# Token tiles loaded from ScalarE's queue, padding issued by two engines, and the last stage's turning and splitting moved to other steps

## What is computed

```python
# stage 1: attention with a threshold, 4 x 8 heads, 576 tokens, head size 64
scores = scale * q @ k.T
scores = where(scores >= max(scores) - tau, scores, -1e9)
x = softmax(scores) @ v                       # 2304 tokens x 512
# stage 2: each token goes to one of 8 experts
logits = x @ w_gate + modality_bias[modality_id]
e = argmax(logits);  gate = softmax(logits)[e]
x = gate * (relu(x @ w1[e]) @ w2[e])          # 512 -> 1024 -> 512
# stage 3: one dense layer with mish
h = x @ w_in                                  # 512 -> 2048
out = (h * tanh(softplus(h))) @ w_out         # 2048 -> 512
```

## Time and profile before

| | |
|---|---|
| median of 3 runs | 1046.27 us (1044.63 to 1048.16) |
| profiled execution: its own time, its span | 1049.75 us, 1048.1 us |
| mean granted clock of TensorE | 0.974 of full |
| PE, PEld, DVE busy | 981.8, 825.5, 673.2 us |
| ACT, POOL busy | 503.7, 466.1 us |
| stage 1 and routing | 0 to about 356 us |
| stage 2 | 356 to 610 us |
| stage 3 | 610 to 1048 us |

### The profile page before, as it was taken

The page is one execution under the profiler, slowest core; times in us unless marked ns, Lnnn a source line. Parts: engine busy times, 40 slices in busy tenths (PEclk is TensorE's granted clock), DMA queues, the critical chain, the costliest instruction groups (busy, mean ns, idle before and its releaser), DMA issues.

```text
span 1048.1 us, 17884 instructions
## 1 busy us (share of the span) xinstructions
PE 981.8 (94%) x6304; PEld 825.5 (79%) x6305; DVE 673.2 (64%) x1200; ACT 503.7 (48%) x952; POOL 466.1 (44%) x558
## 2 busy tenths in 40 slices
PE   6999999999995399999999779999999999999995
PEld 4878877878874288888887668888889888889894
DVE  5788788788785321111115068988879878888773
ACT  3666666666662122222225155554545455545542
POOL 3222235633232663000000027767777777777774
PEclk9999999999998599999999899999999999999998
DMA  2111126122111762111112440000101000000000
GB/s 88 62 51 59 54 90 238 49 90 82 44 50 47 247 206 70 50 40 47 43 40 62 158 121 1 31 1 31 31 31 31 1 31 1 11 21 1 31 1 31
DMA packets 41849, 62.19 MB, mean 59 GB/s; under 512 B 27825, under 2 KB 27825, under 8 KB 41009
## 3 DMA queue, kind: packets, MB, share of 16 engines
q1 hardware_dynamic: 35744, 39.69, 12.2%
q0 software_dynamic: 4480, 18.42, 4.9%
q10 hardware_dynamic: 1552, 3.15, 0.9%
HBM read 43.86 MB, written 17.39 MB: 58 GB/s over the span
## 4 chain that ended last, share of the span: by engine, by line
PE 84%; DVE 6%; DMA 2%; issue 2%; ACT 2%; ACTq 1%; SPq 1%; POOL 1%; POOLq 0%; DVEq 0%
PE psum L369 6%; PE psum L1136 6%; PE psum L1121 6%; PE psum L1119 6%; PE psum L1138 5%; PE psum L1137 5%; PE psum L1120 5%; PE psum L341 4%; DVE rr L1210 3%; PE psum L869 3%; PE psum L845 3%; PE psum L871 3%; PE psum L870 3%; PE psum L847 3%; PE psum L846 3%; PE psum L345 3%
## 5 line engine op out<-in xcount | busy, mean ns | idle before, releaser
L1210 DVE RECIPROCAL rr<-rr 128x384 f32<-128x384 f32 x96 | 244.0, 2542 | 0.9 <-ACT rr L1164 0.9
L1072 POOL TENSOR_TENSOR uu<-uu,ex 128x384 f32<-128x384 f32 x96 | 97.5, 1015 | 291.6 <-ACT uu L1158 291.5
L433 ACT ACTIVATE prob<-ssb,smin 128x576 f32<-128x576 f32 x144 | 111.7, 777 | 112.3 <-DVE ssb L519 112.3
L519 DVE TENSOR_SCALAR_CACHE_REDUCE ssb<-psum,tauk 128x576 f32<-128x576 f32 x144 | 112.7, 816 | 54.6 <-PE psum L328 47.3
L1119 PE MATMUL psum<-x2T_hi,w_in_hi 128*128 128x384 f32 x384 | 132.4, 345 | 5.9 <-DVE gg L1216 3.6
L254 POOL TENSOR_TENSOR limit<-smin,margin 128x2 f32<-128x2 f32 (+1 forms) x80 | 58.2, 727 | 169.3 <-DVE ssb L519 169.1
L1121 PE MATMUL psum<-x2T_hi,w_in_lo 128*128 128x384 f32 x384 | 130.6, 340 | 0.0
L1120 PE MATMUL psum<-x2T_lo,w_in_hi 128*128 128x384 f32 x384 | 130.0, 338 | 0.0
L948 DVE TENSOR_TENSOR hT_lo<-psum,hT_hi 128x512 fp32r<-128x512 f32 x38 | 26.3, 691 | 160.3 <-ACT hT_hi L899 160.3
L1136 PE MATMUL psum<-w_hi,g_hi 128*128 128x512 f32 x288 | 114.7, 398 | 4.3 <-ACT osb L1187 2.5
L1138 PE MATMUL psum<-w_hi,g_lo 128*128 128x512 f32 x288 | 113.8, 395 | 0.0
(11 more groups left out here) (188 smaller groups left out, 2236.2 us busy)
## 6 DMA issues: line engine op xcount, KB each, us to landing
qk<-in_qk_dram SPq DMA_DIRECT2D x16, 640.0 KB, 4.0
vsb<-in_v_dram SPq DMA_DIRECT2D x16, 384.0 KB, 3.3
xrow<-xs SPq DMA_DIRECT2D x21, 256.0 KB, 3.0
ys<-ysb SPq DMA_DIRECT2D x19, 257.0 KB, 3.0
stage<-in_w_in_dram POOLq DMA_DIRECT2D x16, 256.0 KB, 3.6
wa<-in_wa_dram SPq DMA_DIRECT2D x2, 2048.0 KB, 8.8
wb<-in_wb_dram SPq DMA_DIRECT2D x2, 2048.0 KB, 11.1
yrow<-ys SPq DMA_DIRECT2D x5, 771.0 KB, 4.6
```

The source lines that it names most:

```text
L433: act.activation(prob[:, n % 3, cols], ssb[:, w, cols], ACT.Exp, bias=smin[:, w, h:h + 1], scale=-1.0).then_inc(exp_done, 1)
L519: dve.tensor_scalar(ssb[:, w, h * S:(h + 1) * S].rearrange("p (a q) -> p a q", a=2), b_bank if h else a_bank, factor, BIG, ALU.mult, ALU.m ...
L1210: dve.reciprocal(rr[:, n % 4], rr[:, n % 4]).then_inc(r_done, 1)
```

## The change

1. Padding: ACT writes the zeros behind experts 0, 2, 4 and 6, SP those behind 1, 3, 5 and 7.
2. `load_x` is issued by ACT: tiles 0 and 1 before `x_hi(0)`, tile i+2 at the end of ACT's part of tile i. SP is left with `wa`, `wb`, `store_y` and its share of the padding, and no longer waits for `scattered` and `padded`.
3. The gates and numbers have a semaphore of their own, `aux_in`. PE waits for `xrow` alone; ACT's `previous_y(i)` waits for the gates of tiles up to i+1, where it waited for everything up to i.
4. `counts` stands before `turn_x(0)` on PE, before `x_hi(0)` on ACT, before `x_lo(0)` on DVE.
5. In stage 3, `TURN` is [10, 11, 13, 14] for [3, 5, 7, 9]; the splitting of `w_out` is at steps 2, 4, 6 and 8 for 0, 2, 4 and 6; the next chunk's numbers are read at step 12 for 10.
6. `up`, at the first step of a chunk, waits for each quarter of the turned rows before its own three matmuls, where it waited for all four before the first.
7. The last `down` of a chunk raises `col_done` after each output bank, and `out_copy` waits for its bank alone.

```diff
@@ attention_phase, scalar
         act.wait_ge(ends_known, 1)
-        for e in range(E):
+        for e in range(0, E, 2):
             row = act.value_load(tab["ends"][0:1, e:e + 1], min_val=e * CAP, max_val=e * CAP + N)
             act.dma_start(io["xs"][bass.ds(row, P), :], t["zrow"][:]).then_inc(t["padded"], 16)
@@ expert_phase
+    def load_x(eng, i):
+
+        row = eng.value_load(tab["rows"][0:1, 0, bass.ds(i, 1)], min_val=0, max_val=E * CAP - P)
+        if not (isinstance(i, int) and i == 0):
+            eng.wait_ge(x_turned, i)
+        src = io["xs"][bass.ds(row, P), :]
+        eng.dma_start(xrow[:].rearrange("p (h d) -> p h d", h=H),
+                      src.rearrange("p (h c) -> p h c", h=H)[:, :, 0:D]).then_inc(x_in, 16)
+        if not (isinstance(i, int) and i < YRING):
+            eng.wait_ge(y_stored, 16 * (i + 1))
+        eng.dma_start(ysb[:, bass.ds(i % YRING, 1), DM:YW],
+                      src[:, GATE_COL:ID_COL + 1]).then_inc(aux_in, 16)
+
     def sync(sp):
+        sp.sem_inc(y_stored, 16 * YRING)
+        sp.wait_ge(t["ends_known"], 1)
+        for e in range(1, E, 2):
+            row = sp.value_load(tab["ends"][0:1, e:e + 1], min_val=e * CAP, max_val=e * CAP + N)
+            sp.dma_start(io["xs"][bass.ds(row, P), :], t["zrow"][:]).then_inc(t["padded"], 16)
+        sp.wait_ge(tables, 2)
         tiles, ranks = counts(sp)
...
-        sp.sem_inc(y_stored, 16 * YRING)
-        sp.wait_ge(scattered, 16 * TT * B)
-        sp.wait_ge(t["padded"], 16 * E)
-        load_x(0)
-        load_x(1)
-        sp.wait_ge(tables, 2)
         with sp.Fori(0, ranks) as r:
...
             with sp.Fori(first, end) as i:
-                load_x(i + 2)
                 store_y(i)
@@ expert_phase, tensor
-            pe.wait_ge(x_in, 32 * i + 32)
+            pe.wait_ge(x_in, 16 * i + 16)
...
-        turn_x(0)
         pe.wait_ge(tables, 2)
         tiles, ranks = counts(pe)
+        turn_x(0)
@@ expert_phase, scalar
             act.wait_ge(down_done, i + 1)
-            act.wait_ge(x_in, 32 * i + 32)
+            act.wait_ge(aux_in, 16 * i + 32)
...
-        x_hi(0)
         act.wait_ge(tables, 2)
         tiles, ranks = counts(act)
+        act.wait_ge(scattered, 16 * TT * B)
+        act.wait_ge(t["padded"], 16 * E)
+        load_x(act, 0)
+        load_x(act, 1)
+        x_hi(0)
...
                 h_hi(i, 1)
+                load_x(act, i + 2)
@@ mish_phase
-    TURN = [3, 5, 7, 9]
+    TURN = [10, 11, 13, 14]
...
-            if isinstance(c, int) and c == 0 and n < 2 * WP and n % 2 == 0:
-                op(n // 2)
+            if 2 <= n < 2 + 2 * WP and n % 2 == 0:
+                op(n // 2 - 1)
@@ mish_phase, tensor
-            if f == 0:
-                pe.wait_ge(x2_out, KT * (chunk + 1))
...
             for k in range(KT):
+                if f == 0:
+                    pe.wait_ge(x2_out, KT * chunk + k + 1)
...
-            last.then_inc(down_done, 1)
+                if f == FT2 - 1:
+                    last.then_inc(col_done, 1)
+            if f < FT2 - 1:
+                last.then_inc(down_done, 1)
@@ mish_phase, scalar
             if n % FT2 == FT2 - 1:
-                act.wait_ge(down_done, g + 1)
...
                 for j in range(CT):
+                    act.wait_ge(col_done, chunk * CT + j + 1)
                     act.copy(osb[:, j], out_bank[j]).then_inc(out_ready, 1)
@@ mish_phase, vector
-            if n % FT2 == TURN[-1] + 1 and not (isinstance(c, int) and chunk >= NCH):
+            if n % FT2 == TURN[-1] - 2 and not (isinstance(c, int) and chunk >= NCH):
```

More of the change, by code:

```diff
@@ L182, in attention_phase @@
     split_own = sem("split_own")
-    ends_known = sem("ends_known")
+    ends_known = t["ends_known"]
     a_bank, b_bank = psum[:, 0:2, 0:HALF], psum[:, 2:4, 0:HALF]
@@ L737, in expert_phase @@
     x_in, y_out, y_stored, up_done, down_done = (t[n] for n in ("x_in", "y_out", "y_stored", "up_done", "down_done"))
-    w_in_done, x_out = t["w_in_done"], t["x_out"]
+    w_in_done, x_out, aux_in = t["w_in_done"], t["x_out"], t["aux_in"]
     w1_hi_done = sem("w1_hi_done")
@@ L788, in gpsimd @@
                 load_stage(p + 2)
-    def sync(sp):
-        tiles, ranks = counts(sp)
[L793 to L803, removed]
+    def load_x(eng, i):
[9 more added lines that the diff above has]
+                      src[:, GATE_COL:ID_COL + 1]).then_inc(aux_in, 16)
+    def sync(sp):
+        sp.sem_inc(y_stored, 16 * YRING)
[4 more added lines that the diff above has]
+        sp.wait_ge(tables, 2)
+        tiles, ranks = counts(sp)
         def store_y(i):
@@ L935, in scalar @@
         previous_y(tiles)
-        act.wait_ge(x_in, 32 * tiles + 64)
+        act.wait_ge(x_in, 16 * tiles + 32)
+        act.wait_ge(aux_in, 16 * tiles + 32)
     def vector(dve):
@@ L950, in h_lo @@
                               ALU.subtract).then_inc(h_out, 1)
+        tiles, ranks = counts(dve)
         x_lo(0)
-        tiles, ranks = counts(dve)
         with dve.Fori(0, ranks) as r:
@@ L1002, in mish_phase @@
     down_done = sem("down2_done")
+    col_done = sem("col_done")
     out_ready = sem("out_ready")
@@ L1168, in g_high @@
             act.wait_ge(g_done, g + 1)
-            behind(act, down_done, c, n, 4)
+            if g >= 4:
+                before = g - 3
+                act.wait_ge(down_done, before - before // FT2)
+                if before % FT2 == 0:
+                    act.wait_ge(col_done, before // FT2 * CT)
             act.copy(g_hi[:, n % 4], gg[:, n % 2]).then_inc(g_hi_done, 1)
@@ L1173, in x_high @@
             act.wait_ge(turned, c * KT + k + 1)
+            if c == 1 and k == 0:
+                act.wait_ge(w2_ready, WP * ranks + WP)
             act.copy(xT_hi[w][:, k], x_bank(c, k)).then_inc(x_hi_done, 1)
@@ L1303, in build @@
         for name in ("padded", "w1_next", "w2_next", "w1_in", "w2_in", "w1_ready", "w2_ready", "w2_hi_done", "tables", "scattered", "x_in", "x_out",
-                     "y_out", "y_stored", "w_in_done"):
+                     "y_out", "y_stored", "w_in_done", "ends_known", "aux_in"):
             t[name] = sem(name)
```

## The result

The changed kernel takes **1050.52 us** (median of 6 runs, 1049.95 to 1052.04); beside it the kernel before took 1046.85 (1044.63 to 1048.16). The ratio is 1.0038, 95% interval 1.0024 to 1.0052: **slower by 3.7 us**, where 1041.4 was forecast and the range ended at 1046.5. The profiled execution took 1050.41, its span is 1048.7.

The account below looks back on a forecast made before the run. PE was taken to bound the kernel, with DVE setting the pace in the last stage's chunk 0. Terms summed to -4.8 us from the profiled 1049.75, giving 1044.9; less 3.5 to the median, 1041.4 us, range 1033.5 to 1046.5.

Parts of the forecast that it names:

- the base: The profiled execution of the kernel before lay 3.5 us above its median; the same was taken off the changed kernel.
- The start: Start of stage 2: tile 0's rows land behind `wa` and `x_hi(0)` behind tile 1's issues, +1.7 us.
- chunk ends: Last stage: `x_high` leaves the chain before the copy `down` waits for, in 4 of 5 changes, -1.5 us.
- chunk 0: First chunk of the last stage, paced by DVE: moved splittings and turnings let `up(16)` end earlier, -3.3 us.
- change of rank: Between ranks in stage 2: `load_x(17)` on ACT delays the copies of `wa` and so PE, +2.0 us.
- tile 18: Stage 2: its rows still end with the weights, so PE's stall ends at the same place, -0.1 us.
- end of stage 2: `x2T_lo` begins some 1.3 us later, but PE starts after the first quarter, 1.4 to 1.5 earlier: -0.2 us.
- tail: Kernel's end: the first of three copies starts two banks earlier, POOL's scatters hide the rest, -1.4 us.
- Each tile: Stage 2: ACT's 2.1 us for issuing rows fit in its 7.12 us of idle time, hidden 19 times.
- Rival 4: Gain is not there: weights delay tiles 0, 2, 18 by their upper bounds, chunk 0 gives 1.5; 1044 to 1050, chance 0.2.
- Rivals 1 and 2: Tile 18's rows escape the weights, 1035.1, chance 0.12; a queue of its own is quick, 1030.8, chance 0.13.
- rival 3: Stage 2: ACT is late for every tile, `load_x` taking over 7.1 us; 1058 if 8 us, chance 0.05.

Follow-up runs that it names:

- r_before: A second profiled execution of the kernel before, nothing changed: 1047.48 us, beside a median of 1047.23.
- r_moves_only: The kernel before with only the last stage's turnings, weight splittings and reading of numbers moved to other steps: 1046.53 us against 1047.12, ratio 0.9994.
- r_hold_start: Changed kernel, SP's weight loads held in every rank until rows landed, POOL's `stage` loads too, `x_hi(0)` before `load_x(1)`: 1038.91 us, ratio 0.9916.
- r_small_pieces: Changed kernel with each of SP's weight loads issued as 16 DMAs with pieces of 1 KB instead of 16 KB: 1040.17 us, ratio 0.9935.
- r_pad_one: Changed kernel with all eight paddings issued by ACT, none by SP: 1051.14 us, ratio 1.0042.

## Why the prediction was wrong

Four steps failed. The largest, 3.6 us, is the base: I took the excess of one execution off the changed kernel too. The start was mis-sized by 2.7, the chunk ends were forecast as a gain of 1.5 and cost 0.6, and chunk 0 gave 1.0 less. Its terms, against the marks of the two profiles:

| step of the prediction | forecast | measured |
|---|---|---|
| start (first up matmul, 359.78 before) | +1.7 | +4.4 |
| change of rank (wait at `wa`'s copies) | +2.0 | +1.9 |
| tile 18, with the 2.0 inside | -0.1 | +0.4 |
| end of stage 2 | -0.2 | -1.2 |
| chunk 0 | -3.3 | -2.3 |
| chunk ends | -1.5 | +0.6 |
| tail | -1.4 | -1.3 |
| sum, between profiled executions | -4.8 | +0.6 |
| from the profile to the median | -3.5 | +0.1 |

- **The start, right mechanism, mis-sized.** Everything that the rows wait for had landed at 349.25 (forecast 349.3, though the last was a token scatter and not the padding), `wa` left at 349.32 (forecast 348 to 349), the rows came 1.4 us behind the end of `wa` (forecast 1.2), `x_hi` behind `load_x(1)` cost 0.4 (forecast 0.3). The sum took 348.3 for the issue of `wa` and its 9.0 us from an undisturbed load, and then left out the 1.2 us that it had just named: 348.3 + 9.0 + 1.2 is 358.5, not 357.5. Measured, 349.32 + 9.3 + 1.4 is 360.1. Of the 2.6 us, 1.0 is the later issue of `wa`, 0.3 its own time and nearly all the rest the slip. The bound of +4 that I had put on this was just passed. Where rows end with the weights, each us that the weights slip is a us for PE.
- **Each tile, right.** ACT's issues are hidden: `relu` still waits 7.12 us for PE.
- **Change of rank, right.** From `relu(15, 0)` to the copies of `wa` it is 564.87 - 557.67 = 7.20 us, before 558.30 - 553.01 = 5.29.
- **Tile 18, right in its place, short by 0.5.** The lead was 0.6 us (forecast 0.8). The turning at 592.07, less the start's 4.4, is 587.7 (forecast 587.3). The rows landed at 578.19 + 13.8 = 592.0, just behind `wb` (the gates hang on the same end), although over half of the packets of ACT's queue, 632 of 1,184, had passed by 583. Behind the turning PE's first matmul came 1.22 us later for 0.77 (593.29; before 588.45): ACT's `previous_y(17)`, which `down(17)` waits for, got its gates only then and ran at 592.55. So tile 18's first `up` is 4.87 us late, the start's 4.4 and 0.4 more (601.82 for 596.95).
- **End of stage 2, right as far as it went; the other execution's clock did the rest.** DVE begins `x2T_lo` at 618.10 for 611.58, 1.65 us later than the 4.87 account for (forecast 1.3), and PE starts 0.70 us behind it where it took 2.10 (-1.4, forecast -1.4 to -1.5). That leaves -1.5. It is in the profile of before: there the first `up` took 3.84 us (613.68 to 617.52), in the changed kernel 2.36. PE, and its window with the granted clock, of before and of `r_before`, then PE of the changed kernel:

```profile
613.68 0.41 PE L1119 MATMUL psum<-x2T_hi,w_in_hi 128*128 128x384 f32 x1 [1.97 <-DVE x2T_lo L1220]
613.00:617.00 4.00, 3.32 (x12) 3.35 (x13) 0.61 (x3) 0.00 (x0) 0.00 (x0) 0.64 0.96 276
```

```profile
612.81 0.41 PE L1119 MATMUL psum<-x2T_hi,w_in_hi 128*128 128x384 f32 x1 [1.94 <-DVE x2T_lo L1220]
613.00:617.00 4.00, 4.00 (x24) 4.00 (x24) 0.56 (x1) 1.15 (x3) 0.02 (x1) 1.00 0.97 331
```

```profile
618.80 0.41 PE L1126 MATMUL psum<-x2T_hi,w_in_hi 128*128 128x384 f32 x1 [0.35 <-DVE x2T_lo L1236]
```

- **Chunk 0, mis-sized by 1.0.** The mechanism is borne out by `r_moves_only` (-1.97); the waits alone give nothing here (80.15 beside 80.14 of before), and the last 0.35 comes only with both. Some 0.6 of the missing us is a wait that the sum did not have: with turnings at neighbouring steps PE stands for DVE's `x2T_lo` of the one before (two waits in chunk 0, 0.6 us, none before), as at 679.55, behind which it is busy up to the 20th clamp. One edit to ACT is not in the list of changes: it waits for the last `w_low` before it rounds the next chunk's first quarter. That was long done (657.5 for 664.6).

```profile
PE psum L1115 <- DVE x2T_lo L1236: 0.6, 2, 0.4
```

- **Chunk ends, wrong.** I took `x_high` out of ACT's chain and counted 0.38 per change for it. The turning itself (0.35 on PE) leaves the same step, so that PE also comes to `down` sooner; and behind it POOL's three scatters stand ahead of `g_lo`, which now sets the end. Of the wait for `osb` 0.3 went in four changes, the wait for `g_lo` grew by 1.0: a cost of 0.16 per change where a gain of 0.38 was forecast.
- **From profile to median, wrong.** I subtracted the 3.5 us by which the profiled execution of before lay above its median, as if every execution had that excess. It has places, where the granted clock comes back behind a wait. The second profiled execution of the same kernel is 0.2 us ahead at the first `up`, 1.1 at the first `up` of tile 18 (595.86 for 596.95), behind the stall of that tile, and 2.35 at the first clamp (615.17 for 617.52). The last step is the 1.5 us shown above: a wait of 1.97 us with a granted clock of 0.64 behind it in the one, a wait of 1.94 with 1.00 in the other. I had expected the difference in one place, at tile 18. The changed kernel's profiled execution has a full clock there (its first `up` takes 2.36 us), so it has no such excess to take off; the kernel's executions lie within 2.1 us of each other and its profiled one 0.1 below the median. What decides in a single execution whether the clock falls is open; `r_hold_start` has the last stage as changed and 0.64 in 606 to 610.

The errors are 2.7 + 0.5 - 1.0 + 1.0 + 2.1 + 0.1 = 5.4; with 3.6 for the base that is 9.0 of the 9.1 us. The 3.6 and the -1.0 belong together: both hold the 1.5 us of clock in the profile of before. Rival 4 (the gain is not there, 1044 to 1050) came nearest, though 1050.5 is just above it: its bound of +4 at tile 0 was nearly met, while tile 18 and chunk 0 stayed far from theirs. Rivals 1 and 2 fell with the 10.1 and 13.8 us of the rows, rival 3 with the 7.12.

## What to carry to other kernels

A queue also keeps an order. Before a small load that something waits for is moved to a queue of its own, look at which large load stood behind it: freed from the queue, the large one needs a wait of its own (two waits were worth 11 us here), or smaller pieces (1 KB for 16 KB gave 10 us). When a step leaves an engine's chain, look whether another engine loses time at the same step, and what stands next in line. And before a profile's distance from the median is carried over to the changed kernel, ask where it arises; a second profiled execution tells.

## What the runs showed of the hardware

- Two queues with work on the same DMA engines pass piece for piece in some stretches, whatever the size: 122 pieces of 256 bytes beside 121 of up to 16 KB in 583 to 587. In others they don't: 265 beside 16 in 580.5 to 581.5, where the small ones had started first, and 765 beside 154 of 1 KB in `r_small_pieces`.
- 256 KB in pieces of 256 bytes took 3.1 us alone, 5.2 beside two `stage` loads, 6.3 beside those and pieces of 1 KB, and 10.1 to 13.8 beside pieces of 16 KB.
- With two engines issuing the padding the last token scatter took 7.31 us to land, with one (`r_pad_one`) 5.0, from 341.71 to the end of POOL's wait for it at 346.72; the padding, issued within 4.9 us, then landed before it and no longer set the time.
- A wait of nearly the same length had a full clock behind it in one execution of a kernel and not in another (1.94 us and 1.00, 1.97 us and 0.64, both in 613 to 617). In `r_hold_start` a stall of 1.9 us, in place of two of 0.5, was followed by 0.64 in 367 to 371.
